# Attention and two MLPs on one core: down-sampled keys split 128 and 16 instead of 72 and 72, and weight preparation in other periods

## The reference, cut to what matters

```python
def _attn_ref(q, k, v):                      # (4, 8, 576, 64) each
    q_d, k_d, v_d = (mean over 4 neighbouring rows)   # 144 rows
    out_up = np.repeat(sm_attn(q_d, k_d, v_d), 4, axis=2)
    mask = np.abs(pos[:, None] - pos[None, :]) < 4
    out_local = softmax(where(mask, scale * q @ k.T, -1e9)) @ v
    return out_up + out_local

x = attention as (2304, 512)
h = x @ w_in;  x = (h - np.tanh(h)) @ w_out           # 512 -> 2048 -> 512
x = (sigmoid(x @ w_gate) * (x @ w_val)) @ w_out2      # 512 -> 1536 -> 512
```

## Time and profile before

| | |
|---|---|
| median of 3 runs | 920.0 us (919.44 to 920.88) |
| profiled execution | 921.94 us, of which the span (first to last instruction) is 920.1 us |
| TensorE busy (matmul) | 887.6 us, 96% of the span |
| VectorE / ScalarE / GpSimd busy | 584.3 / 381.2 / 286.9 us |
| mean granted clock of TensorE | 0.993 of full speed |
| chain that ended last | 83% TensorE |

### The profile page before, as it was taken

One profiled execution on the slowest core, in us unless ns is written; L12 is line 12 of the kernel. 1 busy time (PEld: TensorE's weight loads), 2 busy tenths in 40 slices (PEclk: granted clock), 3 DMA queues, 4 the chain that ended last, 5 costly groups with the idle time before them and its releaser, 6 DMA issues.

```text
span 920.1 us, 15648 instructions
## 1 busy us (share of the span) xinstructions
PE 887.6 (96%) x6088; PEld 836.1 (91%) x6088; DVE 584.3 (63%) x922; ACT 381.2 (41%) x720; POOL 286.9 (31%) x234
## 2 busy tenths in 40 slices
PE   6989989998999999999998999999999999999997
PEld 4877789998999999999997899999999999999996
DVE  7898865657866568656587556566544456544445
ACT  4676854544423234323253643544222243222221
POOL 4878865773111001030017756712200001000000
PEclk9999999999999999999999999999999999999999
DMA  8896576659645354545232877679665555665511
GB/s 242 223 219 169 192 274 236 258 192 379 250 151 223 144 220 148 213 163 205 93 109 89 341 287 279 271 267 381 265 251 206 206 206 206 237 244 206 206 47 68
DMA packets 35817, 197.01 MB, mean 214 GB/s; under 512 B 3392, under 2 KB 4928, under 8 KB 22688
## 3 DMA queue, kind: packets, MB, share of 16 engines
q1 hardware_dynamic: 29072, 161.64, 48.1%
q0 software_dynamic: 4032, 29.36, 8.3%
q10 hardware_dynamic: 2640, 5.01, 2.1%
HBM read 139.90 MB, written 56.10 MB: 213 GB/s over the span
## 4 chain that ended last, share of the span: by engine, by line
PE 83%; POOL 4%; issue 4%; DVE 4%; DMA 2%; ACT 2%; SPq 0%; ACTq 0%; DVEq 0%; POOLq 0%
PE banks L819 43%; PE banks L891 18%; PE banks L1007 16%; PE banks L765 1%; DMA mid_raw<-in_moe_w_out_dram 1%; PE banks L793 1%; POOL win L599 1%; PE banks L739 1%; PE banks L750 1%; DVE x_op L1374 1%; PE banks L782 1%; DMA v_four<-in_v_dram 1%; POOL mid L613 1%; POOL win_raw L587 0%; PE banks L810 0%
## 5 line engine op out<-in xcount | busy, mean ns | idle before, releaser
L819 PE MATMUL banks<-x_op,pair 128*128 128x384 f32 x1512 | 276.9, 335 | 1.7 <-DVE cg_sum L1561 1.7
L819 PEld LDWEIGHTS banks<-x_op,pair 128*128 128x128 f32 x1512 | 265.1, 188 | 9.7 <-DVE cg_sum L1561 2.1
L891 PE MATMUL banks<-g_parts,mid 128*128 128x384 f32 x1152 | 227.3, 336 | 4.3 <-DVE x_all L1466 4.1
L819 PE MATMUL banks<-x_op,win 128*128 128x384 f32 x1008 | 204.0, 338 | 6.2 <-ACT c_sum L1121 5.1
L891 PEld LDWEIGHTS banks<-g_parts,mid 128*128 128x128 f32 x1152 | 203.0, 189 | 5.9 <-DVE x_all L1466 5.9
L819 PEld LDWEIGHTS banks<-x_op,win 128*128 128x128 f32 x1008 | 178.7, 190 | 7.6 <-ACT c_sum L1121 5.7
L1007 PE MATMUL banks<-wout,p_parts 128*128 128x512 f32 x648 | 163.5, 393 | 1.7 <-issue 1.7
L1466 DVE TENSOR_TENSOR x_all<-banks,x_all 128x384 f32<-128x384 f32 x168 | 92.7, 556 | 83.0 <-PE banks L891 82.6
L1007 PEld LDWEIGHTS banks<-wout,p_parts 128*128 128x128 f32 x648 | 120.3, 188 | 22.6 <-issue 2.1
L1586 DVE TENSOR_TENSOR x_all<-banks,x_all 128x512 f32<-128x512 f32 x90 | 62.2, 691 | 113.6 <-PE banks L1007 113.6
L626 POOL DMA_DIRECT2D wout<-kept_out x12 | 6.5, 540 | 211.4 <-PE banks L1007 211.4
(11 more groups left out here) (99 smaller groups left out, 993.3 us busy)
## 6 DMA issues: line engine op xcount, KB each, us to landing
pair<-kept_pair SPq DMA_DIRECT2D x24, 1792.0 KB, 10.8
win<-kept_in SPq DMA_DIRECT2D x16, 1792.0 KB, 7.3
kept_pair<-pair SPq DMA_DIRECT2D x12, 1792.0 KB, 11.6
mid<-kept_mid POOLq DMA_DIRECT2D x16, 1024.0 KB, 5.1
kept_in<-win SPq DMA_DIRECT2D x8, 1792.0 KB, 6.1
wout<-kept_out POOLq DMA_DIRECT2D x12, 1024.0 KB, 11.8
kept_mid<-mid SPq DMA_DIRECT2D x8, 1024.0 KB, 5.0
kept_out<-wout SPq DMA_DIRECT2D x6, 1024.0 KB, 14.2
```

What stands on the lines that cost most here:

```text
L819: mm = pe.matmul(bk[:, 0:T], weights[:, w, p - 1, kk, :], x_op[:, p - 1, x, kk, :], start=(first and kk == 0 and a == 0), stop=(last and k ...
L891: mm = pe.matmul(bk[:, 0:T], w[:, wp, f, m * P:(m + 1) * P], g[:, gp, 2 * f + t, :], start=(f == 0 and a == 0), stop=(f == 1 and a == 2))
```

## The change

- The 144 down-sampled keys are split as 128 and 16. The 16 lie on partitions 64 to 79 (the second turn takes 80 columns, of which 64 are keys of the first chunk again). `v_four` and `v_down` have 128 partitions. ScalarE's queue loads 128 partitions x 2 KB, and a new `load_v_few` on SP's queue loads the other 16. VectorE clears the second chunk of both buffers at the start.
- On SP `load_v_few(u + 1)` stands in front of `load_qk(u + 3)` and waits for `v_down` of unit u-1. `load_raw(0)` moves from u = 1 to u = 2.
- The warm-up matmuls of TensorE write banks 2, 3 and 4 instead of bank 2 alone.
- GpSimd does the sums of weight block 0 in periods 5 and 6 (4 and 5 before), its four low pieces as two in each of periods 8 and 9 (one each in 8 to 11 before), and the sums of block 1 in 13 and 14 (12 and 13 before). ScalarE's halves of the high parts move one period later with them.
- After the attention GpSimd does `plain_low(0)` before `weight_sums(2)`, and ScalarE does `weight_high(2)` behind `copy_c(1, C21)` instead of ahead of `tanh(0, C11)`.
- VectorE does `local_sum` before the sums and splits over x.

```diff
+    FEW = SD - P
+    KEYS = (slice(0, P), slice(SD - FEW - D, SD))
+    ROWS = (slice(0, P), slice(D, D + FEW))
...
+            def load_v_few(u):
+                wait(sp, s_vd, u - 1)
+                sp.dma_start(v_four[u % 2][ROWS[1], 1, :, :].rearrange("p f n -> p (f n)"),
+                             v_flat[u * P * S + P * FACTOR * P:(u + 1) * P * S].rearrange("(p x) -> p x", p=FEW)).then_inc(s_v4[u % 2], 16)
...
+            sp.wait_ge(s_four, 2)
+            load_v_few(0)
             for u in range(UNITS):
+                if u + 1 < UNITS:
+                    load_v_few(u + 1)
                 if u + 3 < UNITS:
                     load_qk(u + 3)
                 load_v(u)
-                if u == 1:
+                if u == 2:
                     load_raw(0)
...
-                pool.wait_ge(s_v4[u % 2], 16 * (u // 2 + 1))
+                pool.wait_ge(s_v4[u % 2], 32 * (u // 2 + 1))
...
-                if t == 4:
+                if t == 5:
                     weight_sums(0, (0, 1))
-                if t == 5:
+                if t == 6:
                     weight_sums(0, (2, 3))
-                if 8 <= t < 12:
-                    first_weight_low(t - 8)
-                if t == 12:
+                if t == 8:
+                    first_weight_low(0)
+                    first_weight_low(1)
+                if t == 9:
+                    first_weight_low(2)
+                    first_weight_low(3)
+                if t == 13:
                     weight_sums(1, (0, 1))
-                if t == 13:
+                if t == 14:
                     weight_sums(1, (2, 3))
             x_last_sum(0)
-            weight_sums(2)
             pool.wait_ge(s_xlo, splits(0, 4))
             plain_low(0)
+            weight_sums(2)
...
-                    mm = pe.transpose(bk[0:HALF, spot:spot + DROWS], prob_d[u % 3][:, c, hh * HALF:(hh + 1) * HALF],
+                    mm = pe.transpose(bk[0:ROWS[hh].stop, spot:spot + DROWS], prob_d[u % 3][:, c, KEYS[hh]],
...
-                act.dma_start(v_four[u % 2][:, :, :, :].rearrange("p c f n -> p c (f n)"),
-                             v_flat[u * P * S:(u + 1) * P * S].rearrange("(c p x) -> p c x", c=2, p=HALF)).then_inc(s_v4[u % 2], 16)
+                act.dma_start(v_four[u % 2][:, 0, :, :].rearrange("p f n -> p (f n)"),
+                             v_flat[u * P * S:u * P * S + P * FACTOR * P].rearrange("(p x) -> p x", p=P)).then_inc(s_v4[u % 2], 16)
...
-                act.activation(prob_tr[u % 2][:, hh, :], bank[B_R[hh]][0:HALF, 0:REST], ACT.Copy).then_inc(s_cr, 1)
+                rows = slice(0, ROWS[hh].stop)
+                act.activation(prob_tr[u % 2][rows, hh, :], bank[B_R[hh]][rows, 0:REST], ACT.Copy).then_inc(s_cr, 1)
...
                     plain_high(0)
-                    act.wait_ge(s_vd, UNITS)
-                    weight_high(2)
                     tanh(0, C11)
...
-                if 6 <= t < 8:
-                    half_weight_high(0, t - 6)
+                if 7 <= t < 9:
+                    half_weight_high(0, t - 7)
...
-                if t == 14:
+                if t == 15:
                     half_weight_high(1, 0)
...
             copy_c(1, C21)
+            act.wait_ge(s_vd, UNITS)
+            weight_high(2)
             plain_high(1)
```

More of the change, by code:

```diff
@@ L187, in attention_and_mlps @@
         early = Room(RING + 2 * WIN_BYTES, RING + 2 * WIN_BYTES + 4 * WS)
-        v_four = [room.tile(f"v_four{i}", [HALF, 2, FACTOR, P]) for i, room in enumerate((low, early))]
-        v_down = [low.tile(f"v_down{i}", [HALF, 2, P]) for i in range(2)]
+        v_four = [room.tile(f"v_four{i}", [P, 2, FACTOR, P]) for i, room in enumerate((low, early))]
+        v_down = [low.tile(f"v_down{i}", [P, 2, P]) for i in range(2)]
         prob_d = [room.tile(f"prob_d{i}", [DROWS, 3, SD]) for i, room in enumerate((low, low, early))]
@@ L193, in attention_and_mlps @@
         REST = HALF + 3 * DROWS
-        prob_tr = [room.tile(f"prob_tr{i}", [HALF, 2, REST]) for i, room in enumerate((sums, low))]
+        prob_tr = [room.tile(f"prob_tr{i}", [P, 2, REST]) for i, room in enumerate((sums, low))]
         ident = low.tile("ident", [P, P])
@@ L219, in attention_and_mlps @@
         s_zeros = sem("zeros_ready")
+        s_four = sem("v_four_cleared")
         s_band = sem("band_ready")
@@ L720, in _ @@
             pe.wait_ge(s_zeros, 1)
-            for _ in range(8):
-                pe.matmul(down[:, :], zeros_b[:, 0:P], zeros_b[:, :], start=True, stop=True)
+            for b in (2, *B_R, 2, *B_R, 2, 2):
+                pe.matmul(bank[b][:, :], zeros_b[:, 0:P], zeros_b[:, :], start=True, stop=True)
             pe.wait_ge(s_const, 2)
@@ L802, in turned_down @@
             def turned_down(u, c, hh):
-                return prob_tr[u % 2][:, c, HALF:REST].rearrange("p (n q) -> p n q", n=3)[:, :, hh * D:hh * D + THIRD]
+                return prob_tr[u % 2][ROWS[c], c, HALF:REST].rearrange("p (n q) -> p n q", n=3)[:, :, hh * D:hh * D + THIRD]
             def down_values(u):
@@ L809, in down_values @@
                     for hh in range(2):
-                        mm = pe.matmul(values_out[hh * D:(hh + 1) * D, S:S + SD], v_down[u % 2][:, c, hh * D:(hh + 1) * D],
+                        mm = pe.matmul(values_out[hh * D:(hh + 1) * D, S:S + SD], v_down[u % 2][ROWS[c], c, hh * D:(hh + 1) * D],
                                        turned_down(u, c, hh), start=(c == 0), stop=(c == 1),
@@ L1386, in _ @@
             dve.memset(zeros_b[:, :], 0.0).then_inc(s_zeros, 1)
+            for i in range(2):
+                dve.memset(v_four[i][:, 1, :, :], 0.0).then_inc(s_four, 1)
             for i in range(3):
@@ L1410, in _ @@
                     averages(t + 1)
+                if t < UNITS:
+                    local_sum(t)
                 if 10 <= t < 13:
@@ L1414, in _ @@
                     x_low(0, (1, 7)[t - 13])
-                if t < UNITS:
-                    local_sum(t)
                 if t == UNITS:
```

## The result

The changed kernel takes 911.89 us (median of 5 runs, 910.69 to 913.55) against 919.44 us before (5 runs, 917.88 to 920.88): a ratio of 0.9919, with a 95% interval of 0.9902 to 0.9936. Its profiled execution took 912.11 us, of which the span is 910.3. The forecast was 909.5, with a range of 904.5 to 916.5: a gain of 10.5 us, of which 7.5 came.

A forecast was written before the change was run, and what follows sets the result against it. TensorE and VectorE were taken as full in undisturbed attention periods, with losses from late instruction packets, half clock and the first quad's wait. Terms summed to -10.5 us: 911.4 profiled, 909.5 median, range 904.5 to 916.5.

The forecast's parts named there:

- VectorE's order: VectorE's sum over x, placed behind `local_sum`, should meet GpSimd's work less: -0.8 us, ends 0 and -1.4.
- Start: GpSimd waits 7.58 us for the first `v_four`, which should land earlier: -0.5 us, ends 0 and -1.3.
- First gap: TensorE's 2.85 us gap in the stretch from 13.73 us: earlier instruction packet, -3.9 us, ends 0 and -4.65.
- Moved block 0: Raw block 0, loaded a round later, must still be moved in later attention periods: +1.0 us, ends 0 and 2.3.
- Second gap: TensorE's 3.38 us gap in the stretch from 55.59 us: less queue backlog, -2.4 us, ends 0 and -5.1.
- the rival of 905.0: In the attention, both instruction gaps vanish and the moved block costs nothing: 15 us off, chance 0.14.
- GpSimd's two low pieces: Two low pieces in one period, 8 and 9, delay `normalise`, on which TensorE's turns wait: +0.5 us, ends 0 and 2.3.
- a sign of being wrong: A new wait of TensorE for `v_down` or GpSimd's `normalise` in periods 8 to 10; no size given.
- First quad: After the attention, ScalarE's tanh chain starts earlier; TensorE's 2.53 us gap and clock loss go: -4.4 us, ends -1.5 and -4.5.
- The turns' wider weight load: The first chunk's three turns load 128 columns of weights instead of 72: taken as 0, ends 0 and 3.4 us.
- SP is held: `load_v_few`'s wait for `v_down` delays SP's loads of q, k and windows: 14 us over 13 periods, 923.5, chance 0.08.
- just shift: The quads behind the first run at ScalarE's and TensorE's own pace, so they only move earlier; no time priced.

The follow-up runs named there:

- experiment 7: The kernel before, unchanged, measured and profiled once more: 917.91 us, ratio 0.999.
- experiment 11: The changed kernel with GpSimd's low pieces of the first weight back to one in each of periods 8 to 11: 908.58 us, ratio 0.9893.
- experiment 9: The eighth with block 0's load one period later, as in the changed kernel: 906.6 us, ratio 0.9866.
- the eighth: The kernel before with only the 128/16 split, the first quad's new order and the last 16 keys' matmuls reading 80 rows: 907.38 us, ratio 0.987.
- experiment 12: The changed kernel with the last 16 keys on partitions 0 to 15 instead of 64 to 79: 911.99 us, ratio 0.9925.
- experiment 10: The eighth with `local_sum` ahead of VectorE's sums and splits of the weights, as in the changed kernel: 906.86 us, ratio 0.9871.
- experiment 1: The kernel before with only the split of the down-sampled keys into 128 and 16: 913.18 us, ratio 0.9931.
- experiment 3: The kernel before with only the first quad's order: `plain_low(0)` ahead of `weight_sums(2)`, `weight_high(2)` behind `copy_c(1, C21)`: 914.28 us, ratio 0.9939.
- experiment 4: The changed kernel with the matmuls over the last 16 keys reading 80 rows, zeros in the lower 64: 909.08 us, ratio 0.9895.
- experiment 2: The kernel before with each unit's transfer of 72 partitions issued as two, of 64 and 8, on the same queue: 924.08 us, ratio 1.0033.
- experiment 6: The changed kernel with the down-sampled keys back in two halves of 72, all other edits kept: 917.12 us, ratio 0.9975.
- 5: The changed kernel with the first weights' sums, low pieces and ScalarE's halves back in the periods of before: 909.1 us, ratio 0.9885.

## Why the prediction came out right, step by step

The time was forecast 2.4 us too low and the gain 3.0 us too large. The mechanism of the first quad held, and both gaps went, though not for the reason given. That the sum came so near is in part luck: three terms (the moved block, the low pieces, VectorE's order) were off by 0.8 to 2 us each and partly cancel, the 16-row matmuls, priced at 0, cost 1.2 us, and the two gaps were priced from one execution, of which a second one (experiment 7) shows the first at less than half and the second not at all. The steps:

**Start, -0.5.** The turns of period 1 begin at 13.09 instead of 13.73: -0.6. Right. They begin behind a wait for GpSimd in both traces, 1.77 us now and 2.16 before; only in the changed kernel's trace does the clock fall behind it (at 14 us), so that the first of the three periods takes 7.04 us.

**First gap, -3.9.** The gap is gone, and the stretch of three periods gave 2.67 us. The term was too large by 1.2: 0.4 of it is the longer period, the rest the half clock. It still comes once, now behind the wait for GpSimd: 17.93 less 3 x 5.45 is 1.6 us, where 0.75 had been left. This half clock does not belong to the change: experiment 11 runs the same program up to period 8, has no fall here, and takes 10.89 us for the first two periods instead of 12.49.

**Moved block 0, +1.0.** The prediction held that the block loads the queues of the later periods. It costs nothing: experiment 9 is 0.8 us faster than the eighth by the medians, which is no difference by their intervals.

**Second gap, -2.4.** The gap of 3.38 is gone whole, as the rival of 905.0 said; its time did not come, for the reasons in the next terms. Only 1.82 us came out of the stretch, because the next term took its place.

**GpSimd's two low pieces, +0.5 (0 to 2.3).** This is the term that was mis-sized. The prediction laid the extra piece against the wait of 1.66 us for `v_four` in period 8. That wait is gone too, but the pieces then waited 1.47 us for ScalarE's half, which moved with them. TensorE waits 0.81 and 0.99 us, a wait for `normalise` in periods 8 to 10 that the prediction had named as a sign of being wrong. Experiment 11 measures the doubling at 2.5 us by the traces, just outside the ends given. The clock, half for 3.4 us in after's trace, is not the reason (experiment 12).

**VectorE's order, -0.8.** The wrong sign: +0.6 in its stretch by experiment 10, nothing in the time. The sum of the earlier trace rows that took 2.42 us takes 0.97 in the changed kernel (at 73.74), as the prediction hoped, but 1.00 us in experiment 1 too (at 68.51), where VectorE's order and the low pieces are those of before: so the order was not needed for it. The sum one period earlier takes 2.82 us at 65.64, for 2.60 before (at 67.05) and 1.47 with one piece a period (experiment 11, at 63.22): the pairing costs VectorE 1.35 us there. Why VectorE as a whole loses 0.62 us by the order was not followed further.

**First quad, -4.4.** 15.89 to 11.55 us from the start of the matmuls to the mark: -4.3, and the whole stretch of the earlier trace rows 17.98 to 13.63, -4.35. Experiment 3 shows 4.2 us with these two lines alone. Right to 0.2 us, against a trace in which the clock fell behind the wait; in experiment 7, the same kernel, 1.6 us of it were not there to gain.

**The turns' wider weight load, 0.** Right: the three turns of 128 columns take 0.45 us, as the three of 80 columns after them, in after's trace. By the Trainium skill ("TensorE: Matmul & The Clock Gate", LDWEIGHTS) they would cost 107 ns each for their columns, an estimate from that page; the records have a mean of 142 ns for them, more than the rule, and yet nothing of it reaches the path, since the loads lie beside the matmuls. What costs 0.15 us a period came from the matmuls of `down_values` instead, of which the prediction said that they "move the same columns". They do, but the 16-row ones have a mean of 304 ns in the stretch, those of 128 rows 286. Experiments 4 and 12 settle it. Two side sums are slightly off, and nothing hangs on them: the page's estimate for 48 turns is 2.2 us instead of 2.3, and the two clears without cover would be 1.3 us by 503 ns for 384 columns, not 1.

**What the split works by.** Here the prediction's reason failed, though the gain came. It read the gaps as the instruction packet being late behind queues in which 12 engines carried `v_four`, and priced 16 engines at 7% less on each. Experiment 2 gave the load 16 engines and lost 3.0 to 4.2 us. The runs show instead that with the 128 and 16 all transfers take less engine time for their bytes: 0.78 of the time at 236 GB/s from 12 to 65 us (experiment 1: 0.83 at 252), against 0.90 at 225 before (experiments 3 and 7: 0.92 at 227, 0.91 at 223). That is 3.3 thousandths a GB/s instead of 4.0, 17% less, where the prediction counted 7% fewer packets on the loaded engines. With it GpSimd's waits for `v_four` after the first go from 8 to 9 us in five times (11.7 in six in experiment 6) to none (after, 5, 8, 9 and 10) or one of 0.6 to 1.5 us (1, 4, 11 and 12). In four traces with 72 partitions in one piece TensorE has gaps by "issue" in three; in nine traces with the split up to 104 us there is a single one (0.88 us, experiment 4). That these gaps are late instruction packets, as the prediction read them, is borne out by the starts of the packets (experiment 7); that the packets are late because of the data in the queues is still inferred. Their sum is not fixed: 6.6 us in before's trace, 2.6 in its second, none in experiment 3, where TensorE waits 4.6 us for GpSimd instead.

What stays open is why a transfer over 72 partitions makes the bytes of all queues dearer, or, if not the number 72, what in it does: two rows of each partition in one transfer, or the queue it stands in. The split changed all of these together, and experiment 2 only rules the number of engines out. One more thing came with the split and was not tested alone: the wait of `load_v_few` for `v_down` holds SP's queue. From 12 to 65 us SP waits there 18.9 us in nine times in the changed kernel, so that q, k and the windows are issued at other moments than before. Spacing the loads may itself be what eases the queues. As the rival "SP is held" it did no harm: from 10 to 105 us neither TensorE nor VectorE waits for a load of q or k there.

**From the mark to the end** the changed kernel takes 788.32 us, before 787.75 (after and then before):

```profile
121.98:910.30 788.32, 775.68 (x4225) 744.45 (x4224) 473.75 (x758) 294.45 (x483) 190.88 (x141) 1.00 0.57 215
```

```profile
132.35:920.10 787.75, 774.32 (x4225) 743.16 (x4224) 472.69 (x757) 294.41 (x481) 189.23 (x137) 1.00 0.56 214
```

The work is the same, and the prediction's "just shift" holds but for the clock. The changed kernel has half clock twice in it (PEclk 0.66 in both windows); experiment 10, with 786.68 us, in neither place:

```profile
208.00:213.00 5.00, 3.70 (x13) 3.71 (x14) 3.83 (x3) 4.31 (x8) 2.36 (x1) 0.66 1.00 423
485.00:490.00 5.00, 5.00 (x21) 4.61 (x20) 3.51 (x4) 0.00 (x0) 4.92 (x6) 0.66 0.00 0
```

## What to carry to other kernels

Look at how much engine time a byte costs (the DMA share over the GB/s of the same window), not at the share alone: the split, with its new wait on SP, moved that by 17% for all queues together, and the waits it fed showed up on GpSimd and TensorE. When a gap reads "issue", profile the same kernel twice before pricing it; the one of 3.38 us was not there the second time. Look also for the last instruction packet ahead of its end. Before pairing two pieces of background work in one period, ask what both of them wait for: here the pairing cost 2.5 us, more than its waits of 1.8 us at TensorE. And compare stretches long enough to let a loss come back: 3.3 us over three periods were 2.5 over eight.

## What the runs showed of the hardware that was not expected

A matmul over 16 rows behind one over 128 costs more than one over 80: the mean is 304 to 306 ns against 286, and the eight matmuls of `down_values` take 0.81 instead of 0.66 us. In the records of the changed kernel the first weight load of 16 rows starts 0.21 us after the matmul ahead of it started (25.18 behind 24.97 us); with 80 rows (experiment 4) it follows at 0.12 (23.62 behind 23.50). Reading 80 rows, with zeros under the 16, removed it.

One and the same wait is followed by the half clock in one execution and not in the next. In the changed kernel VectorE ends a wait of TensorE of 2.11 us at 484.46, and the clock is at 1.2 GHz from about 485.6 us; experiment 10 has the same wait and keeps 2.4 GHz. Of fourteen traces four have the fall behind this wait (after, 1, 6 and 9) and ten do not:

```profile
484.46 5.83 PE L913 MATMUL banks<-g_parts,mid 128*128 128x384 f32 x22 [2.11 <-DVE x_all L1494]
```

```profile
479.83 2.38 PE L905 MATMUL banks<-g_parts,mid 128*128 128x384 f32 x12 [2.12 <-DVE x_all L1485]
```

Falls in the last 5 us left aside, traces without one take 786.2 and 786.7 us from the mark to the end (experiments 3 and 10), those with one 787.0 to 787.9 (6, before, 8 and 11), those with two 788.3 to 789.6 (after, 1, 4, 5, 9 and 12): about 1 us each, which is as much as several of the prediction's terms. Experiments 2 and 7, whose first fall lasts twice as long, take 789.95 and 791.3.
